# A sparse expert layer: the next tile's rows turned behind the upper block of the expert rows instead of ahead of it

## The chip, the cores and the metric

The kernel runs on one core of a Trainium2 chip. The metric is the device time of one execution in microseconds (us); three runs were timed. One further execution was profiled, and all rows below are from it.

## The reference

Three layers follow one another on 1536 tokens of 512 values: a bucketed attention, a dense mixture of experts, and a sparse mixture of experts. The change touches the third alone. There each token goes to the one expert whose embedding fits best, and its row is scaled by the probability of that choice:

```python
logits = xn @ en.T / tau
expert_idx = np.argmax(logits, axis=1)
probs = softmax(logits)
gate_w = probs[np.arange(N), expert_idx]
for e in range(E):                      # E = 8
    mask = expert_idx == e
    h = np.maximum(x[mask] @ w1[e], 0.0)        # 512 -> 1024
    out[mask] = gate_w[mask, None] * (h @ w2[e])  # 1024 -> 512
```

## The kernel before

Every fp32 operand of a large product is kept as two parts: a rounded one ("hi") and the rest ("lo"). matmul_x3 makes a product from three matmuls, hi by lo, hi by hi and lo by hi (lines L478, L479, L480). A cast on ScalarE makes hi, a subtraction on VectorE makes lo.

The sparse layer works in tiles of up to 128 tokens of one expert. A loop with a count known only at run time (tiles2) runs over the tiles of each expert, and the experts follow in order; tile numbers run through. Each engine has its own copy of this loop, written out by hand, and works strictly in its written order; semaphores alone tie the engines together. There is no scheduler.

What happens for tile i, by names of the code:

- GpSimd gathers the token rows into x_row (L656) and later stores y_row by a list of rows (L665). The gather for a later tile waits until PE has turned the x_row before it (s_xrow_t).
- PE, turn_row (L1104): four 128x128 transposes of x_row into PSUM bank 2. ScalarE, x_hi (L1341), then VectorE, x_lo (L1836), split the bank. They are done one tile ahead, for tile i + 1.
- PE, up part: for each of two column blocks c of 512, 12 matmuls into bank c. VectorE's relu (L1861) writes block c of g_row. turn_h(i, c) (L1113) turns it by four transposes into bank 6 + c; ScalarE's copy (L1361) makes g_hi of it, VectorE's g_lo (L1865) the rest. The lower block is c = 0, the upper one c = 1. turn_h(i, 0) stands inside the up part of c = 1.
- PE, down part: for f = 0 to 7, three matmuls into bank 4; f below 4 needs the lower block of g, f from 4 on the upper.
- ScalarE's y_tile (L1351) scales bank 4 into y_row.

Beside this the weights of the next expert are split: w2_hi2 (L1294) and w2_lo (L1726, called "second" in the loop) in each tile of the expert, w1_hi2 (L1289) and w1_lo2 (L1720) behind its last tile. SP loads weights when the raw buffers are free.

Of the kernel before, what the change touches and what calls it, by code (L numbers as in the profile page):

```python
# [27 lines left out]
def program(nc, q, k, v, proj, w_gate, w1, w2, emb, tau, m2w1, m2w2, out):  # L28
# [8 lines left out]
    KD, KF = DM // P, FF // P  # L37
# [14 lines left out]
    def place(name, shape, dt, at=None):  # L52
        size = 2 if dt == BF16 else 4
        for n in shape[1:]:
            size *= n
        here = top if at is None else at
        t = nc.alloc_sbuf_tensor_at(name, shape, dt, offset=here[0])
        here[0] += (size + 31) // 32 * 32
        assert here[0] <= nc.sbuf_usable_end, name
        return t  # L60
# [80 lines left out]
    w2_raw_of = [place("w2_raw_even", [P, KF, DM], F32, small), w2_raw]  # L141
# [334 lines left out]
    def matmul_x3(pe, acc, a, b, start, stop):  # L476

        pe.matmul(acc, a[0], b[1], start=start, stop=False)  # L478
        pe.matmul(acc, a[0], b[0], start=False, stop=False)  # L479
        return pe.matmul(acc, a[1], b[0], start=False, stop=stop)  # L480
# [233 lines left out]
    def _(pe):  # L714
# [385 lines left out]
        def turn_row(i):  # L1100

            pe.wait_ge(s_xrow, 16 * i + 16)
            for kd in range(KD):
                tr = pe.transpose(psum[:, 2, kd * P:(kd + 1) * P], x_row[:, kd * P:(kd + 1) * P], ident[:])  # L1104
            tr.then_inc(s_xrow_t, 1)

        def turn_h(i, c):

            pe.wait_ge(s_relu2, 2 * i + c + 3)
            pe.wait_ge(s_g_lo, 2 * i + c + 1)  # L1110
            for j in range(4):
                f = 4 * c + j
                tr = pe.transpose(psum[:, 6 + c, j * P:(j + 1) * P], g_row[:, f * P:(f + 1) * P], ident[:])  # L1113
            tr.then_inc(s_g_t, 1)

        def tiles2(e, u, first, end, more=True):
            with pe.Fori(first, end) as i:
                pe.wait_ge(s_x_lo, i + 1)
                for c in range(2):
                    pe.wait_ge(s_relu2, 2 * i + c + 1)  # L1120
                    for kd in range(KD):
                        if c == 0:
                            pe.wait_ge(m2.w1_lo, KD * e + kd + 1)
                        if c == 1 and kd == 2:
                            turn_h(i, 0)
                        mm = matmul_x3(pe, psum[:, c, :], [x[:, kd, :] for x in x_s],
                                       [w[:, kd, c * 512:(c + 1) * 512] for w in w1_s], kd == 0, kd == KD - 1)
                    mm.then_inc(s_up2, 1)
                turn_row(i + 1)
                pe.wait_ge(m2.w2_lo, KF * (i + 1) if more else KF * (first + 1))  # L1130
                pe.wait_ge(s_y2, i + 1)
                for f in range(KF):
                    if f % 4 == 0:
                        pe.wait_ge(s_g_lo, 2 * i + f // 4 + 3)
                    if f == 1:
                        turn_h(i, 1)
                    mm = matmul_x3(pe, psum[:, 4, :], [g[:, f, :] for g in g_s], [w[f] for w in w2_p[u]],
                                   f == 0, f == KF - 1)
                mm.then_inc(s_down2, 1)

        tiles2(0, 0, 0, first_end)
        with pe.Fori(0, E // 2 - 1) as e2:
            for u in (1, 0):
                e = 2 * e2 + 2 - u
                tiles2(e, u, *tile_range(pe, e))
        tiles2(E - 1, 1, *tile_range(pe, E - 1), more=False)


    @block.scalar
    def _(act):  # L1150
# [135 lines left out]
        def w1_hi2(e, raw, kds=range(KD)):  # L1286
            act.wait_ge(m2.w1_in, 16 * e + 16)
            for kd in kds:
                act.copy(w1_s[0][:, kd, :], raw[:, kd, :]).then_inc(m2.w1_hi, 1)  # L1289

        def w2_hi2(e, u, raw, fs):
            act.wait_ge(m2.w2_in, 16 * e + 16)
            for f in fs:
                act.copy(w2_p[u][0][f], raw[:, f, :]).then_inc(m2.w2_hi, 1)  # L1294
# [44 lines left out]
        def x_hi(i):  # L1339
            act.wait_ge(s_xrow_t, i + 1)  # L1340
            act.copy(x_s[0][:].rearrange("p k i -> p (k i)"), psum[:, 2, :]).then_inc(s_x_hi, 1)  # L1341
# [5 lines left out]
        def y_tile(i):  # L1347

            act.wait_ge(s_down2, i + 1)
            act.wait_ge(s_y_free, i + 1)  # L1350
            act.activation(y_row[:], psum[:, 4, :], ACT.Copy, scale=p_now[:, 0:1]).then_inc(s_y2, 1)  # L1351

        def tiles2(e, u, first, end, more=True):
            with act.Fori(first, end) as i:
                y_tile(i)
                if more:
                    act.wait_ge(m2.w2_lo, KF * (i + 1))
                    w2_hi2(e + 1, 1 - u, w2_raw_of[1 - u], range(0, KF - 1))
                for c in range(2):
                    act.wait_ge(s_g_t, 2 * i + c + 1)  # L1360
                    act.copy(g_s[0][:, 4 * c:4 * c + 4, :].rearrange("p f i -> p (f i)"),  # L1361
                             psum[:, 6 + c, :]).then_inc(s_g_hi, 1)
                    if c == 0:
                        if more:
                            w2_hi2(e + 1, 1 - u, w2_raw_of[1 - u], (KF - 1,))
                        x_hi(i + 1)
            if more:
                w1_hi2(e + 1, w1_raw_of[1 - u])

# [4 lines left out]
        first_end = act.value_load(start_i[0:1, 1:2], min_val=1, max_val=SLOTS)  # L1374
        act.wait_ge(s_x_lo, 1)
        tiles2(0, 0, 0, first_end)
        with act.Fori(0, E // 2 - 1) as e2:
            for u in (1, 0):
                e = 2 * e2 + 2 - u
                tiles2(e, u, *tile_range(act, e))  # L1380
        tiles2(E - 1, 1, *tile_range(act, E - 1), more=False)
        every = act.value_load(start_i[0:1, E:E + 1], min_val=E, max_val=SLOTS)
        y_tile(every)
# [3 lines left out]
    def _(dve):  # L1387
# [329 lines left out]
        def w1_lo2(e, raw, kds=range(KD)):  # L1717
            for kd in kds:
                dve.wait_ge(m2.w1_hi, KD * e + kd + 1)
                dve.tensor_tensor(w1_s[1][:, kd, :], raw[:, kd, :], w1_s[0][:, kd, :].bitcast(F32),  # L1720
                                  ALU.subtract).then_inc(m2.w1_lo, 1)

        def w2_lo(done, u, raw, f):

            dve.wait_ge(m2.w2_hi, done + f + 1)
            dve.tensor_tensor(w2_p[u][1][f], raw[:, f, :], w2_p[u][0][f].bitcast(F32), ALU.subtract).then_inc(m2.w2_lo, 1)  # L1726
# [107 lines left out]
        def x_lo(i):  # L1834
            dve.wait_ge(s_x_hi, i + 1)
            dve.tensor_tensor(x_s[1][:].rearrange("p k i -> p (k i)"), psum[:, 2, :],  # L1836
                              x_s[0][:].rearrange("p k i -> p (k i)").bitcast(F32), ALU.subtract).then_inc(s_x_lo, 1)
# [21 lines left out]
        def relu(i, c):  # L1859
            dve.wait_ge(s_up2, 2 * i + c + 1)  # L1860
            dve.tensor_scalar(g_row[:, c * 512:(c + 1) * 512], psum[:, c, :], 0.0, None, ALU.max).then_inc(s_relu2, 1)  # L1861

        def g_lo(i, c):
            dve.wait_ge(s_g_hi, 2 * i + c + 1)
            dve.tensor_tensor(g_s[1][:, 4 * c:4 * c + 4, :].rearrange("p f i -> p (f i)"), psum[:, 6 + c, :],  # L1865
                              g_s[0][:, 4 * c:4 * c + 4, :].rearrange("p f i -> p (f i)").bitcast(F32),
                              ALU.subtract).then_inc(s_g_lo, 1)

        def tiles2(e, u, first, end, more=True):
            with dve.Fori(first, end) as i:  # L1870

                def second(*fs):
                    if more:
                        for f in fs:
                            w2_lo(KF * (i + 1), 1 - u, w2_raw_of[1 - u], f)

                second(0, 1)
                relu(i, 0)
                second(2, 3, 4)
                g_lo(i, 0)  # L1880
                relu(i, 1)
                second(5)
                x_lo(i + 1)
                second(6)
                g_lo(i, 1)
                second(7)
            if more:
                w1_lo2(e + 1, w1_raw_of[1 - u])

        tiles2(0, 0, 0, first_end)  # L1890
        with dve.Fori(0, E // 2 - 1) as e2:
            for u in (1, 0):
                e = 2 * e2 + 2 - u
                tiles2(e, u, *tile_range(dve, e))
        tiles2(E - 1, 1, *tile_range(dve, E - 1), more=False)

    block.__exit__(None, None, None)
# [28 lines left out]
```

## Time and profile before

| | us |
|---|---|
| median of 3 runs | 1570.8 (1570.76 to 1570.91) |
| profiled execution | 1570.51 |
| its span | 1568.6 |
| PE busy | 1545.6 (99%) |
| PE weight loads busy | 1292.6 (82%) |
| VectorE busy | 686.0 (44%) |
| ScalarE busy | 516.0 (33%) |
| GpSimd busy | 332.3 (21%) |

The chain that ended last is PE for 96% of the span. The sparse layer's tiles lie between 1346 and 1560 us. A matmul of 512 columns is listed with some 0.39 us, but the next one starts 0.23 us behind it: matmuls overlap, and their pitch is what counts. PEld rows are the weight loads that go ahead of each matmul. Around each row stand the start, the length, the engine, the line and the tiles, and in brackets the idle time before it with what ended it.

### The profile page before, as it was taken

What the parts mean: (1) busy time and instruction counts of PE and PEld (TensorE: products, weight loads), DVE (VectorE), ACT (ScalarE), POOL (GpSimd) and SP (SyncE); (2) the same over time, 40 slices, a digit from 0 to 9 for tenths busy, and PEclk for the clock granted to TensorE, in tenths of its full rate; (3) what the DMA queues carried; (4) which work ended last, traced back from release to release, by engine and by line L of the source; (5) the groups of instructions that cost most, each with busy time, mean ns of one, the idle gap of its engine ahead of it and who ended that gap; (6) DMA issues with size and microseconds to landing.
All of it is one profiled execution on the core that took longest, in us unless ns stands there. A gap on an engine that the chain in (4) does not pass through costs nothing.

```text
span 1568.6 us, 21673 instructions
## 1 busy us (share of the span) xinstructions
PE 1545.6 (99%) x7493; PEld 1292.6 (82%) x7494; DVE 686.0 (44%) x1242; ACT 516.0 (33%) x946; POOL 332.3 (21%) x563
## 2 busy tenths in 40 slices
PE   8999999999999999999999999999999999999997
PEld 7999997888888888888888888888888888788886
DVE  7999985423222311311322221121132255887665
ACT  6888885012111101101211111011121133676554
POOL 4565656000300300120030030012004000233222
PEclk9999999999999999999999999999999999899999
DMA  6545561101100200110110011011011122774310
GB/s 164 136 113 144 124 179 55 54 1 54 55 1 1 80 27 0 53 53 0 53 54 0 0 68 39 0 53 53 0 38 69 41 81 75 251 260 163 118 40 25
DMA packets 44775, 108.88 MB, mean 69 GB/s; under 512 B 5782, under 2 KB 7830, under 8 KB 44736
## 3 DMA queue, kind: packets, MB, share of 16 engines
q1 hardware_dynamic: 41088, 99.83, 20.4%
q0 software_dynamic: 3424, 8.14, 1.6%
q8 instruction: 24, 0.39, 0.1%
q10 hardware_dynamic: 224, 0.39, 0.1%
q14 instruction: 15, 0.12, 0.0%
HBM read 81.57 MB, written 8.13 MB: 57 GB/s over the span
## 4 chain that ended last, share of the span: by engine, by line
PE 96%; DVE 2%; ACT 1%; issue 1%; POOL 0%; DVEq 0%; POOLq 0%; ACTq 0%
PE psum L478 27%; PE psum L479 26%; PE psum L480 26%; PE psum L786 4%; PE psum L773 2%; PE psum L800 2%; PE psum L799 2%; PE psum L774 2%; PE psum L1113 1%; PE psum L754 1%; PE psum L813 1%; PE psum L920 1%; PE psum L1104 0%; ACT prob L1169 0%; DVE pt_lo L1431 0%
## 5 line engine op out<-in xcount | busy, mean ns | idle before, releaser
L1302 ACT ACTIVATE h_hi<-psum 128x512 fp32r<-128x512 f32 x192 | 114.9, 598 | 878.5 <-PE psum L480 878.5
L478 PE MATMUL psum<-w_lo,h_hi 128*128 128x512 f32 x768 | 304.4, 396 | 0.0
L479 PE MATMUL psum<-w_hi,h_hi 128*128 128x512 f32 x768 | 302.5, 394 | 0.0
L478 PE MATMUL psum<-xt_lo,w_hi 128*128 128x512 f32 x768 | 300.3, 391 | 0.0
L479 PE MATMUL psum<-xt_hi,w_hi 128*128 128x512 f32 x768 | 299.0, 389 | 0.0
L480 PE MATMUL psum<-xt_hi,w_lo 128*128 128x512 f32 x768 | 298.9, 389 | 0.0
L480 PE MATMUL psum<-w_hi,h_lo 128*128 128x512 f32 x768 | 298.5, 389 | 0.0
L1737 DVE SCALAR_TENSOR_TENSOR h_lo<-psum,h_hi 128x512 fp32r<-128x512 f32 x192 | 133.0, 693 | 351.3 <-ACT h_hi L1302 351.3
L1800 DVE SCALAR_TENSOR_TENSOR tok<-psum,route,tok 128x512 f32<-128x512 f32 x83 | 56.8, 745 | 358.6 <-PE psum L480 358.6
L509 POOL CAST w_hi<-w_raw 128x512 fp32r<-128x512 f32 x68 | 41.6, 611 | 802.0 <-PE psum L480 801.6
L480 PEld LDWEIGHTS psum<-w_hi,h_lo 128*128 128x128 f32 x768 | 144.2, 188 | 32.5
L478 PEld LDWEIGHTS psum<-w_lo,h_hi 128*128 128x128 f32 x768 | 144.2, 188 | 32.1
L480 PEld LDWEIGHTS psum<-xt_hi,w_lo 128*128 128x128 f32 x768 | 144.2, 188 | 30.1
L478 PEld LDWEIGHTS psum<-xt_lo,w_hi 128*128 128x128 f32 x768 | 144.2, 188 | 29.8
L479 PEld LDWEIGHTS psum<-xt_hi,w_hi 128*128 128x128 f32 x768 | 144.2, 188 | 29.4
L479 PEld LDWEIGHTS psum<-w_hi,h_hi 128*128 128x128 f32 x768 | 144.6, 188 | 27.4
L1431 DVE TENSOR_TENSOR pt_lo<-psum,pt_hi 128x384 fp32r<-128x384 f32 x192 | 97.5, 549 | 18.4 <-ACT pt_hi L1162 17.7
L1169 ACT ACTIVATE prob<-psum,row_bias,row_scale 128x768 f32<-128x768 f32 x96 | 95.9, 999 | 20.4 <-POOL row_bias L558 18.6
L1441 DVE TENSOR_REDUCE row_min<-psum 128x1 f32<-128x768 f32 x96 | 90.8, 947 | 1.1 <-PE psum L774 0.7
L1162 ACT CAST pt_hi<-psum 128x384 fp32r<-128x384 f32 x192 | 83.0, 486 | 14.1 <-PE psum L786 12.9
L631 POOL TENSOR_TENSOR w_lo<-w_raw,w_hi 128x512 fp32r<-128x512 f32 x64 | 82.6, 1291 | 12.5 <-issue 7.2
L786 PE MATMUL psum<-ident,prob 128*128 128x128 f32 x576 | 80.7, 275 | 2.2 <-DVE pt_lo L1431 1.7
(272 smaller groups left out, 1996.0 us busy)
## 6 DMA issues: line engine op xcount, KB each, us to landing
w_raw<-in_moe_w_dram SPq DMA_DIRECT2D x25, 2048.0 KB, 8.2
w_raw_odd<-in_moe_w_dram SPq DMA_DIRECT2D x4, 2048.0 KB, 10.3
k_hh<-k_hi SPq DMA_DIRECT2D x32, 192.0 KB, 3.0
w_raw_even<-in_moe_w_dram SPq DMA_DIRECT2D x3, 2048.0 KB, 9.2
x_rows<-tok SPq DMA_DIRECT2D x14, 256.0 KB, 2.4
k_raw<-in_k_dram SPq DMA_DIRECT2D x8, 384.0 KB, 3.1
v_raw<-in_v_dram SPq DMA_DIRECT2D x16, 192.0 KB, 3.4
q_b<-q_hi SPq DMA_DIRECT2D x16, 192.0 KB, 4.0
```

The lines of the kernel that those rows point to most:

```text
L478: pe.matmul(acc, a[0], b[1], start=start, stop=False)
L479: pe.matmul(acc, a[0], b[0], start=False, stop=False)
L480: return pe.matmul(acc, a[1], b[0], start=False, stop=stop)
L631: pool.tensor_tensor(w2_s[1][:, f, :], w2_raw[:, f, :], w2_s[0][:, f, :].bitcast(F32), ALU.subtract).then_inc(m1.w2_lo, 1)
L786: tr = pe.transpose(psum[:, 4 + c, j * P:j * P + P], prob[par][:, 3 * c + j, :], ident[:])
L1162: act.copy(pt_hi[half][:, 3 * c:3 * c + 3, a:a + P], psum[:, 4 + c, 0:HALF].rearrange("p (j i) -> p j i", j=3)).then_inc((s_hi_a, s_hi_b)[ ...
L1169: act.activation(prob[t % 2][:].rearrange("p (c j) i -> p c (j i)", c=2), psum[:, score_bank(g, t):score_bank(g, t) + 2, 0:HALF], ACT.Exp, ...
L1302: act.activation(h_s[0][:, f, :], psum[:, f % 4, :], ACT.Relu).then_inc(m1.h_hi, 1)
L1431: dve.tensor_tensor(pt_lo[half][:, 3 * c:3 * c + 3, a:a + P], psum[:, 4 + c, 0:HALF].rearrange("p (j i) -> p j i", j=3), pt_hi[half][:, 3 ...
L1441: dve.tensor_reduce(row_min[:, c], psum[:, score_bank(g, t):score_bank(g, t) + 2, 0:HALF], AX.XY, ALU.min).then_inc(s_min, 1)
L1737: dve.scalar_tensor_tensor(h_s[1][:, f, :], psum[:, f % 4, :], 0.0, h_s[0][:, f, :].bitcast(F32), ALU.max, ALU.subtract).then_inc(m1.h_lo, 1)
L1800: dve.scalar_tensor_tensor(tok[:, tile, 0:DM], psum[:, 4 + i, :], route[:, e, tile:tile + 1], tok[:, tile, 0:DM], ALU.mult, ALU.add).then_ ...
```

## The change

In PE's loop, turn_row(i + 1) goes from between the up part and the down part to behind turn_h(i, 1), which stands behind the three matmuls of f = 0. ScalarE makes x_hi(i + 1) behind the copies of both blocks instead of behind that of the lower one. VectorE makes g_lo(i, 1) before x_lo(i + 1), and second(6) ahead of both. Nothing is added or left out.

```diff
@@ PE, tiles2
                     mm.then_inc(s_up2, 1)
-                turn_row(i + 1)
                 pe.wait_ge(m2.w2_lo, KF * (i + 1) if more else KF * (first + 1))
                 pe.wait_ge(s_y2, i + 1)
                 for f in range(KF):
                     if f % 4 == 0:
                         pe.wait_ge(s_g_lo, 2 * i + f // 4 + 3)
                     if f == 1:
                         turn_h(i, 1)
+                        turn_row(i + 1)
@@ ScalarE, tiles2
                     act.copy(g_s[0][:, 4 * c:4 * c + 4, :].rearrange("p f i -> p (f i)"),
                              psum[:, 6 + c, :]).then_inc(s_g_hi, 1)
-                    if c == 0:
-                        if more:
-                            w2_hi2(e + 1, 1 - u, w2_raw_of[1 - u], (KF - 1,))
-                        x_hi(i + 1)
+                    if c == 0 and more:
+                        w2_hi2(e + 1, 1 - u, w2_raw_of[1 - u], (KF - 1,))
+                x_hi(i + 1)
@@ VectorE, tiles2
                 relu(i, 1)
-                second(5)
+                second(5, 6)
+                g_lo(i, 1)
                 x_lo(i + 1)
-                second(6)
-                g_lo(i, 1)
                 second(7)
```

PE at the end of the up part of a tile (w_hi and w_lo are w1, xt_hi and xt_lo hold w2 here, ISA and REGISTER_ALU prepare a wait), before:

```order
L480 MATMUL psum<-w_hi,x_lo 128x512
L1102 ISA
L1104 MATMUL psum<-ident,x_row 128x128 x4
L1130 REGISTER_ALU
L478 MATMUL psum<-xt_lo,g_hi 128x512
L479 MATMUL psum<-xt_hi,g_hi 128x512
L480 MATMUL psum<-xt_hi,g_lo 128x512
L1109 REGISTER_ALU
L1113 MATMUL psum<-ident,g_row 128x128 x4
L478 MATMUL psum<-xt_lo,g_hi 128x512
```

The same place on PE with the change:

```order
L480 MATMUL psum<-w_hi,x_lo 128x512
L1129 REGISTER_ALU
L478 MATMUL psum<-xt_lo,g_hi 128x512
L479 MATMUL psum<-xt_hi,g_hi 128x512
L480 MATMUL psum<-xt_hi,g_lo 128x512
L1109 REGISTER_ALU
L1113 MATMUL psum<-ident,g_row 128x128 x4
L1102 ISA
L1104 MATMUL psum<-ident,x_row 128x128 x4
L478 MATMUL psum<-xt_lo,g_hi 128x512
```

The four transposes of x_row have moved past three matmuls and past the four transposes of g_row.

VectorE from the upper relu to the end of the tile (L1726 is "second"), before:

```order
L1861 TENSOR_SCALAR g_row<-psum 128x512
L1725 REGISTER_ALU
L1726 TENSOR_TENSOR w_lo<-w_raw,w_hi 128x512
L1835 REGISTER_ALU
L1836 TENSOR_TENSOR x_lo<-psum,x_hi 128x512
L1725 REGISTER_ALU
L1726 TENSOR_TENSOR w_lo<-w_raw,w_hi 128x512
L1865 TENSOR_TENSOR g_lo<-psum,g_hi 128x512
L1725 REGISTER_ALU
L1726 TENSOR_TENSOR w_lo<-w_raw,w_hi 128x512
```

The same place on VectorE with the change (its lines stand one lower in number):

```order
L1860 TENSOR_SCALAR g_row<-psum 128x512
L1724 REGISTER_ALU
L1725 TENSOR_TENSOR w_lo<-w_raw,w_hi 128x512
L1724 REGISTER_ALU
L1725 TENSOR_TENSOR w_lo<-w_raw,w_hi 128x512
L1864 TENSOR_TENSOR g_lo<-psum,g_hi 128x512
L1834 REGISTER_ALU
L1835 TENSOR_TENSOR x_lo<-psum,x_hi 128x512
L1724 REGISTER_ALU
L1725 TENSOR_TENSOR w_lo<-w_raw,w_hi 128x512
```

x_lo has moved behind a w2 rest and g_lo.

## Rows read from the trace of the kernel before

**Rows 1.** Stretches: length, busy us (instructions) per engine, PEclk, DMA share, GB/s.

```profile
1340.00:1346.00 6.00, 4.25 (x21) 3.21 (x21) 3.96 (x20) 2.28 (x4) 0.90 (x5) 0.63 0.63 241
1346.00:1352.00 6.00, 6.00 (x15) 4.69 (x16) 2.97 (x9) 4.59 (x9) 2.40 (x3) 0.52 0.22 54
...
1429.17:1441.52 12.35, 12.35 (x61) 10.19 (x60) 8.12 (x14) 6.60 (x13) 3.32 (x4) 1.00 0.13 43
1441.52:1454.02 12.50, 12.50 (x62) 10.12 (x61) 12.42 (x18) 10.39 (x17) 4.31 (x4) 1.00 0.62 198
```

**Rows 2.** Waits from 1346 us on: who for whom, total us, times, longest.

```profile
POOL x_row L656 <- PE psum L1104: 52.2, 17, 5.1
...
POOL out_dram L665 <- POOL idx_now L509: 3.0, 3, 1.0
...
PEld psum L478 <- DVE w_lo L1720: 2.0, 7, 0.3
...
PE psum L478 <- DVE x_lo L1840: 0.4, 1, 0.4
```

**Rows 3.** Timeline of the weight loads in one tile: start, length, engine, line, operation.

```profile
1429.17 0.59 PEld L1104 LDWEIGHTS psum<-ident,x_row 128*128 128x128 f32 x4
...
1430.08 0.19 PEld L480 LDWEIGHTS psum<-xt_hi,g_lo 128*128 128x128 f32 x1
1430.35 0.56 PEld L1113 LDWEIGHTS psum<-ident,g_row 128*128 128x128 f32 x4
...
1430.98 0.19 PEld L479 LDWEIGHTS psum<-xt_hi,g_hi 128*128 128x128 f32 x1
...
1432.83 0.19 PEld L478 LDWEIGHTS psum<-xt_lo,g_hi 128*128 128x128 f32 x1
```

**Rows 4.** Timeline of PE in the same tile.

```profile
1429.17 0.39 PE L480 MATMUL psum<-w_hi,x_lo 128*128 128x512 f32 x1
1429.40 0.60 PE L1104 MATMUL psum<-ident,x_row 128*128 128x128 f32 x4
...
1430.54 0.60 PE L1113 MATMUL psum<-ident,g_row 128*128 128x128 f32 x4
```

**Rows 5.** Timeline of VectorE in the same tile.

```profile
1428.83 0.69 DVE L1865 TENSOR_TENSOR g_lo<-psum,g_hi 128x512 fp32r<-128x512 f32 x1
1429.60 0.69 DVE L1861 TENSOR_SCALAR g_row<-psum 128x512 f32<-128x512 f32 x1
1430.21 0.68 DVE L1726 TENSOR_TENSOR w_lo<-w_raw,w_hi 128x512 fp32r<-128x512 f32 x1
...
1432.01 0.69 DVE L1865 TENSOR_TENSOR g_lo<-psum,g_hi 128x512 fp32r<-128x512 f32 x1
1432.61 0.68 DVE L1726 TENSOR_TENSOR w_lo<-w_raw,w_hi 128x512 fp32r<-128x512 f32 x1
```

**Rows 6.** All instructions of line L1861: ns shortest/median/longest, first and last start.

```profile
L1861 DVE TENSOR_SCALAR g_row<-psum x34: 678/692/694, 1351.5 to 1553.5; 128x512 f32<-128x512 f32 x34
```

**Rows 7.** Timeline of the weight loads behind a change of the expert.

```profile
1413.04 0.19 PEld L478 LDWEIGHTS psum<-w_lo,x_hi 128*128 128x128 f32 x1 [0.31 <-DVE w_lo L1720]
1413.15 0.19 PEld L479 LDWEIGHTS psum<-w_hi,x_hi 128*128 128x128 f32 x1
1413.39 0.19 PEld L480 LDWEIGHTS psum<-w_hi,x_lo 128*128 128x128 f32 x1
```

**Rows 8.** Timeline of ScalarE in the tile of rows 3.

```profile
1430.04 0.59 ACT L1341 CAST x_hi<-psum 128x512 fp32r<-128x512 f32 x1 [0.72 <-PE psum L1104]
1431.18 0.59 ACT L1361 CAST g_hi<-psum 128x512 fp32r<-128x512 f32 x1 [0.55 <-PE psum L1113]
```

**Rows 9.** Timeline of GpSimd around the change to the third and fourth tile.

```profile
1387.41 0.78 POOL L509 COPY idx_now<-tab 128x3 uint32 x1 [5.37 <-DMA x_row<-x_rows,idx_now]
...
1393.60 0.94 POOL L656 DMA_INDIRECT x_row<-x_rows,idx_now  x1 [1.53 <-PE psum L1104]
```

## The prediction

> **What bounds the kernel now.** I read four views in this order: the table of stretches for two whole tiles of the sparse layer, the table of waits over that layer, the start times on PE, its weight loads, VectorE and ScalarE around one tile's boundary between upper and lower block, and last GpSimd, because the moved step also releases a gather.
>
> PE is busy 12.35 of 12.35 us in one tile and 12.50 of 12.50 in another [rows 1]. From 1346 us on only one wait of PE for another engine is listed, 0.4 us for the first x_lo; its weight loads waited 2.0 us in seven places for L1720 [rows 2]. So the sparse layer is a dense row of PE work. An added PE instruction or wait lengthens it, and other engines matter only when PE reaches something they have not finished.
>
> The place of the change is the end of the up part. Let T0 be the start of its last matmul, 1429.17 [rows 4]. The weight load of turn_row starts at T0 too, its first transpose at 1429.40 = T0+0.23 [rows 3, 4]. VectorE finishes g_lo of the lower half at 1428.83+0.69 = 1429.52 = T0+0.35, and begins relu of the upper half at 1429.60 = T0+0.43, which is done at 1430.29 = T0+1.12 [rows 5]. turn_h(i, 1) needs that relu: its weight load starts at 1430.35 = T0+1.18, 0.06 us after relu's end. Without a wait it would have started one matmul behind the load at 1430.08, at 1430.31 [rows 3]. It is therefore already held back by 0.04 us, which is not seen on PE, since its first transpose runs at 1430.54 = T0+1.37, one matmul pitch (0.23) after 1430.31 [rows 4]. The reader is to see that turn_row lies exactly in the shadow in which relu is made, and that nothing of this shadow is left over. relu takes 678 to 694 ns in all 34 cases [rows 6], so there is no tile in which it is shorter.
>
> **The change part by part.** Nothing is added or removed in count: per tile four transposes, one CAST and one TENSOR_TENSOR change places.
>
> (a) PE. Four transposes keep their price: the weight load of the next matmul stands at 1430.98, the first transpose at 1430.54, so 0.44 us for four, 0.11 each [rows 3, 4]. Behind turn_h they cost 0.44 again. Ahead of it they no longer cost it if the three matmuls of f = 0 could run at once.
>
> They can't. The load of f = 0 would want to start at T0, but it waits for g_lo of the lower half, ready at T0+0.35, so about T0+0.40 (with the 0.06 seen between relu and its waiter, T0+0.41). A late load shows at the change of an expert, where PE waits for L1720: load at 1413.04, the next load (which starts with the late matmul) at 1413.15, the one after at 1413.39 [rows 7]. So the late matmul runs 0.11 us after its load, the second 0.35. The f = 0 matmuls start at T0+0.52, 0.76, 0.99, and turn_h could run at T0+1.22.
>
> relu holds it further. Its end does not move: it hangs on the last up matmul, which stays at T0. The load of turn_h is released at T0+1.18, its first transpose runs at T0+1.29. Then eight transposes at 0.11 end at T0+2.17; before, the matmul of f = 1 came at T0+1.37+0.44 = T0+1.81. Loss: 0.36 us a tile, for 17 tiles (34 relus, two a tile [rows 6]) 6.1 us. Said otherwise: 0.44 moved out of the shadow, less 0.08 because turn_h starts that much sooner.
>
> Bounds of this unknown. A gain is no end of the range, since PE's work stays and it waited for nothing here before. The trace shows no late load of this kind before a transpose. Lower end: if the transpose started at once with its load, the loss would be 0.36-0.11 = 0.25, 4.3 us. Upper end: if it had to wait the full 0.19 of a load, 0.44, and if the two register and wait instructions between turn_h and turn_row, which after a stall are not fetched ahead, cost another 0.06 (the distance from a release to its waiter), 0.50, 8.5 us. I take 0.36, from the only late load in the rows.
>
> The Trainium skill, page "TensorE: Matmul & The Clock Gate", section "Architectural detail: the array is 16× 32×32, not 1× 128×128", says that a matmul can begin before its weight load completes. By that rule the sum stays at 6.1; by a reading in which the load of 0.19 us must be complete it would be 17 x 0.44 = 7.5. The late load of [rows 7] agrees with the rule: 0.11 against 0.19.
>
> (b) The upper half's own chain. g_hi begins 0.64 us behind the first transpose (1430.54 to 1431.18 [rows 4, 8]), now at T0+1.93, done at T0+2.52. g_lo, no longer behind x_lo, starts at T0+2.57 instead of 1432.01 = T0+2.84 [rows 5] and is done at T0+3.26. PE's load for f = 4 stood at 1432.83 = T0+3.66 [rows 3] against g_lo's end at T0+3.53; it moves to T0+4.02. The slack grows from 0.13 to 0.76 us, worth nothing, as PE was not waiting there: at 1432.83 the load runs on time.
>
> (c) The x chain. x_hi follows g_hi on ScalarE, done about T0+3.1; x_lo starts one VectorE pitch (1429.60 to 1430.21, 0.6 us [rows 5]) behind g_lo, at T0+3.17, and ends at T0+3.86. The next tile needs it about T0+6.8 (21 matmuls at a pitch of 0.23 behind T0+2.17, less a pitch by which the load is ahead). Hidden by three microseconds of down matmuls. Without that cover each late 0.1 would cost 0.1.
>
> (d) The change of an expert. The fourth rest w_lo of the next w1 was too late in seven places (2.0 us of waiting loads [rows 2]); in time each costs 0.15 us (a tile of 12.50 instead of 12.35 [rows 1]), 1.0 us in all. VectorE reaches these rests one pitch behind its last w2 rest, which stood at 1432.61 = T0+3.44 [rows 5] and now stands at T0+3.77: 0.33 later, while PE comes 0.36 later. Gain 0.03 each, 0.2 us. w1_hi moves 0.5 to 0.6 us later on ScalarE but stays ahead of VectorE.
>
> (e) GpSimd. The gather of the next rows waits for turn_row: 52.2 us of waiting in 17 cases [rows 2]. turn_row starts at T0+1.73 instead of T0+0.23, so the gather goes 1.5 us later. Hidden behind the same wait, with what stands under the third rival. SP's loads follow w_lo and move by 0.3.
>
> Sum: 6.1-0.2 = +5.9 us against the profiled execution's 1570.51 (span 1568.6), so 1576.4. The median of the runs is 1570.8, 0.3 above; forecast 1576.7, +0.38%. Changes within 0.2% (3.1 us) can't be told from none.
>
> **Rivals.**
> Not slower: PE finds relu ready. Were turn_h's load really held by PE's own order and the 0.04 us a chance, the transposes would only change places, and instead the late w_lo at the expert changes would be all that moves: PE's 7 x 0.15 = 1.0 us may go, 1569.8. It decides in this way if turn_h's load can start by T0+0.80. For it speaks that no row names relu as releaser of PE. Against: relu ends at T0+1.12 and starts with the last matmul's result, 0.43 behind T0. Chance 0.06.
>
> The clock falls. PE would now stand idle 0.36 us in each tile. In 1340 to 1346 us, with PE busy 4.25 of 6, the granted clock was 0.63, and 0.52, nearly all of it at the lower level of 1.2 GHz, in the 6 us behind, where 15 matmuls ran in 6.0 us, 2.6 us more than at a pitch of 0.23 [rows 1]. One more such stretch gives 1579.3, one in each tile 1621. Against: the idle share would be 3%, not 29%. Chance 0.03. The Trainium skill, "TensorE: Matmul & The Clock Gate", section "A second HAM failure mode: psum-queue depth-cycling", says that frequent micro-idles between groups of matmuls can make the clock oscillate; no row here shows it at idle gaps this short.
>
> GpSimd becomes late. Where weights are being loaded, the gathered rows kept the next step waiting 5.37 us, and the gather of the next tile then waited only 1.53 for PE [rows 9]; in three tiles the store went straight behind idx_now [rows 2]. 1.5 us more makes store, p_now and y_row of these tiles late; ScalarE does y_row, seven casts and then g_hi, so PE would wait for g_lo. If 1 us of it reached PE in three tiles, 1579.7. Against: after a delay of 1.5 the next gather's release is 1.5 later too. Chance 0.07.
>
> **Chances.** Forecast 0.82 (its own range 1574.9 to 1579.1 from the bounds in (a)), not slower 0.06, clock 0.03, GpSimd 0.07, else 0.02. Range 1574.3 to 1579.9, which reaches from a little below the forecast's range to the GpSimd case. Faster by over 0.2%: 0.02; within: 0.07; slower: 0.91.
>
> **What would show it.** Tiles of 12.71 and about 12.83 us instead of 12.35 and 12.50; two listed waits of PE's loads per tile, for g_lo L1864 and relu L1860; turn_h's load 0.06 us behind relu's end; eight transposes in a row at 0.11; g_lo at T0+2.57. I am wrong if the load of f = 0 starts at T0, if turn_h's starts before T0+1.1, or if a tile grows by under 0.25 or over 0.50 us.

## The result and the profile after

Six runs of the changed kernel have a median of 1576.99 us (1576.77 to 1578.34), six of the kernel before on the same chip 1570.92 (1570.76 to 1571.13): 6.07 us more, ratio 1.004 with a 95% interval of 1.0029 to 1.005. The forecast was 1576.7. The profiled span is 1575.0 us against 1568.6.

To keep the sparse layer apart from what runs ahead of it, I take T0 (the start of the last up matmul) of the first and of the last of its 17 tiles from the timelines: 1354.48 and 1553.08 before, 1354.73 and 1559.14 after. The 16 tiles between them take 198.60 and 204.41 us, so 5.81 more or 0.363 a tile. The same loss behind the last T0 makes 6.2; the other 0.25 of the span's 6.4 lies ahead of the first T0, where nothing was changed. In the profiles of all kernels below the first T0 lies anywhere between 1353.21 and 1355.92, so the 16 tiles tell small differences better than the run times.

The stretches of two tiles, one in the middle of an expert and one behind a change of expert, with length, busy us per engine in the order PE, PEld, VectorE, ScalarE, GpSimd, granted clock, DMA share and GB/s:

```profile
1380.42:1393.29 12.87, 12.71 (x62) 10.08 (x60) 12.51 (x18) 10.29 (x17) 3.79 (x4) 1.00 0.96 366
1482.72:1495.41 12.69, 12.59 (x61) 10.11 (x60) 8.20 (x14) 6.50 (x13) 3.32 (x4) 1.00 0.13 41
```

Where PE was busy for the whole tile before [rows 1], it now is not, and the granted clock stays at 1.00. The idle time is smaller than the loss, because the row of a matmul is listed with 0.39 us while its pitch is 0.23. Waits in the sparse layer of the changed kernel, as who for whom, us in all, times, longest:

```profile
POOL x_row L656 <- PE psum L1104: 62.6, 14, 4.8
POOL x_row L656 <- DMA out_dram<-y_row,idx_now: 14.4, 3, 4.9
...
PEld psum L478 <- issue: 8.2, 16, 0.6
...
PEld psum L1113 <- DVE g_row L1860: 2.0, 11, 0.2
PEld psum L478 <- DVE w_lo L1719: 1.7, 7, 0.2
PEld psum L478 <- DVE xt_lo L1725: 1.4, 2, 0.7
PE psum L478 <- DVE g_lo L1864: 1.1, 5, 0.3
```

Of the waits of PE and its loads in this list [rows 2] had only the one for w_lo, of 2.0 us. The new ones have to be read with the code beside them: "issue" (but for one of 0.4 us that the kernel before had as well) and "xt_lo" both stand at the first load of f = 0, which the code lets wait for the lower g_lo. The view names no releaser, or the wrong one, because that g_lo had ended 0.12 us before the load began. One tile shows it; first the weight loads (start, length, engine, line):

```profile
1431.45 0.19 PEld L480 LDWEIGHTS psum<-w_hi,x_lo 128*128 128x128 f32 x1
1432.15 0.19 PEld L478 LDWEIGHTS psum<-xt_lo,g_hi 128*128 128x128 f32 x1 [0.51 <-issue]
1432.26 0.19 PEld L479 LDWEIGHTS psum<-xt_hi,g_hi 128*128 128x128 f32 x1
1432.50 0.19 PEld L480 LDWEIGHTS psum<-xt_hi,g_lo 128*128 128x128 f32 x1
1432.85 0.47 PEld L1113 LDWEIGHTS psum<-ident,g_row 128*128 128x128 f32 x4 [0.17 <-DVE g_row L1860]
1433.29 0.47 PEld L1104 LDWEIGHTS psum<-ident,x_row 128*128 128x128 f32 x4
...
1433.83 0.19 PEld L479 LDWEIGHTS psum<-xt_hi,g_hi 128*128 128x128 f32 x1
...
1435.68 0.19 PEld L478 LDWEIGHTS psum<-xt_lo,g_hi 128*128 128x128 f32 x1
```

PE in the same tile:

```profile
1431.68 0.39 PE L480 MATMUL psum<-w_hi,x_lo 128*128 128x512 f32 x1
1432.18 0.47 PE L478 MATMUL psum<-xt_lo,g_hi 128*128 128x512 f32 x1
1432.49 0.39 PE L479 MATMUL psum<-xt_hi,g_hi 128*128 128x512 f32 x1
...
1432.96 0.60 PE L1113 MATMUL psum<-ident,g_row 128*128 128x128 f32 x4
1433.39 0.60 PE L1104 MATMUL psum<-ident,x_row 128*128 128x128 f32 x4
```

VectorE:

```profile
1431.34 0.69 DVE L1864 TENSOR_TENSOR g_lo<-psum,g_hi 128x512 fp32r<-128x512 f32 x1
1432.10 0.69 DVE L1860 TENSOR_SCALAR g_row<-psum 128x512 f32<-128x512 f32 x1
1432.71 1.28 DVE L1725 TENSOR_TENSOR w_lo<-w_raw,w_hi 128x512 fp32r<-128x512 f32 x2
1434.21 0.69 DVE L1864 TENSOR_TENSOR g_lo<-psum,g_hi 128x512 fp32r<-128x512 f32 x1 [0.22 <-ACT g_hi L1361]
1434.82 0.68 DVE L1835 TENSOR_TENSOR x_lo<-psum,x_hi 128x512 fp32r<-128x512 f32 x1
1435.42 0.68 DVE L1725 TENSOR_TENSOR w_lo<-w_raw,w_hi 128x512 fp32r<-128x512 f32 x1
```

Here T0 is 1431.68. The lower g_lo ends at T0+0.35, as before, and relu at T0+1.11, as before [rows 5]: neither has moved. PE has: its f = 0 load waits until T0+0.47, turn_h's until T0+1.17, and the load behind f = 1's first matmul comes at T0+2.15, where it came at T0+1.81 [rows 3]. turn_h starts 0.09 us sooner than before [rows 4], and 0.43 to 0.44 of turn_row now follow it.

Two loads wait in this tile, but only one of the waits holds PE. The first transpose of turn_h, 1432.96, stands 0.47 us behind the second matmul of f = 0, 1432.49. That is two pitches of 0.23, as in a row without a gap. In all 17 tiles this distance is 0.46 to 0.48, in the 11 where a wait for relu is listed and in the 6 where none is. So turn_h's load waited for relu while PE still had matmuls to run, and the lower g_lo alone sets the time.

### The profile page after: what moved, and what is told of

It is laid out like the page before. It is cut to its first block, busy times and chain, and to the rows that moved or that the text cites. A ratio compares the mean times of both kernels' runs of the same rounds, so it can differ in the third digit from the quotient of the medians.

```text
span 1575.0 us, 21673 instructions
## 1 busy us (share of the span) xinstructions
PE 1549.4 (98%) x7493; PEld 1291.4 (82%) x7494; DVE 687.2 (44%) x1242; ACT 514.2 (33%) x946; POOL 329.9 (21%) x563
## 4 chain that ended last, share of the span: by engine, by line
PE 93%; DVE 3%; issue 2%; ACT 1%; DVEq 0%; DMA 0%; POOL 0%; ACTq 0%; POOLq 0%
PE psum L478 26%; PE psum L479 25%; PE psum L480 25%; PE psum L786 4%; PE psum L773 2%; PE psum L800 2%; PE psum L799 2%; PE psum L774 2%; PE psum L1113 1%; PE psum L754 1%; PE psum L813 1%; PE psum L920 1%; DVE xt_lo L1725 0%; DVE w_lo L1725 0%; PE psum L1104 0%
```

## The experiments

All times are medians beside runs of the kernel before on the same chip, whose median there was 1569.5 to 1571.1. "16 tiles" is the stretch from the first T0 to the last, "tile" the common distance of two T0 within an expert and over a change of expert, all from the timelines.

| kernel | time (before) | ratio, 95% interval | 16 tiles | tile within / at a change |
|---|---|---|---|---|
| before | | | 198.60 | 12.34 / 12.50 |
| changed | 1576.99 (1570.92) | 1.0040 (1.0029 to 1.0050) | 204.41 | 12.69 / 12.79 to 12.90 |
| PE's move alone | 1591.25 (1571.05) | 1.0129 (1.0112 to 1.0146) | 218.57 | 13.51 / 13.85 |
| ScalarE and VectorE alone | 1573.11 (1571.05) | 1.0014 (1.0005 to 1.0024) | 201.60 | 12.35 / 12.89 |
| changed, filler in the old place | 1578.15 (1571.05) | 1.0048 (1.0032 to 1.0065) | 205.64 | 12.80 / 12.89 |
| before, one transpose of four | 1570.33 (1571.05) | 0.9995 (0.9985 to 1.0005) | 198.16 | 12.26 / 12.51 |
| before, filler behind turn_row | 1577.22 (1571.13) | 1.0041 (1.0025 to 1.0056) | 204.62 | 12.78 / 12.79 |
| changed, turns behind f = 1 | 1582.19 (1571.13) | 1.0074 (1.0059 to 1.0089) | 209.28 | 12.70 / 13.50 |
| before, w1_lo last | 1570.55 (1571.13) | 0.9997 (0.9988 to 1.0006) | 198.17 | 12.35 / 12.35 |
| changed, lower turn earlier | 1577.50 (1569.47) | 1.0043 (1.0027 to 1.0060) | 204.25 | 12.66 / 12.76 to 12.92 |
| both earlier | 1582.03 (1569.47) | 1.0076 (1.0059 to 1.0093) | 208.70 | 12.66 / 13.26 to 13.61 |
| lower rest freed | 1577.97 (1570.78), one run | | 205.55 | 12.65 / 13.10 |
| both freed | 1576.02 (1570.78), one run | | 205.01 | 12.46 / 13.25 |

**The two halves of the change.** PE's move alone:

```diff
-                turn_row(i + 1)
...
                     if f == 1:
                         turn_h(i, 1)
+                        turn_row(i + 1)
```

> The kernel before with PE's part of the change alone: turn_row behind turn_h(i, 1), while ScalarE still makes x_hi before the upper g_hi and VectorE x_lo before the upper g_lo. Theory (the shadow of relu and of the lower g_lo is lost): 0.36 us a tile as in the whole change, and on top the upper g_lo comes late: x_hi from T0+2.35, x_lo 2.99, a w2 rest 3.59, g_lo 4.19 to 4.88, PE's load for f = 4 at T0+4.93 instead of 4.02, 0.79 more a tile; tiles of about 13.5 us, some 21 us over before, about 1592. Rival (the order on ScalarE and VectorE is worth nothing, PE alone decides): as the whole change, 1577.

Measured 1591.25 and tiles of 13.51. Waits of that kernel:

```profile
PEld psum L478 <- DVE g_lo L1865: 15.6, 17, 1.0
...
PE psum L478 <- DVE g_lo L1865: 8.4, 16, 0.5
```

The upper g_lo (L1865) is now waited for by PE's load of f = 4 in every tile. The theory's term for it holds (12.70+0.79 = 13.49). So the new order on ScalarE and VectorE is worth some 14 us to this PE order, though it saves nothing against the kernel before.

The change on ScalarE and VectorE alone, with turn_row in its old place:

```diff
-                    if c == 0:
-                        if more:
-                            w2_hi2(e + 1, 1 - u, w2_raw_of[1 - u], (KF - 1,))
-                        x_hi(i + 1)
+                    if c == 0 and more:
+                        w2_hi2(e + 1, 1 - u, w2_raw_of[1 - u], (KF - 1,))
+                x_hi(i + 1)
...
-                second(5)
-                x_lo(i + 1)
-                second(6)
-                g_lo(i, 1)
+                second(5, 6)
+                g_lo(i, 1)
+                x_lo(i + 1)
```

> The change on ScalarE and VectorE alone, PE's order as before. Theory: PE's stretch at the block boundary stays at 12.34 us a tile, since turn_row fills the shadow again; but VectorE now idles until the upper g_hi is done and reaches the rests of the next w1 at T0+4.45 instead of T0+4.03, so each of the seven late changes of an expert costs 0.42 us more: 1573.8. Rival 1 (the loss of the whole change lies in these two engines): 1577. Rival 2 (their order is worth nothing): 1570.9.

Tiles within an expert stay at 12.35, but for two of 12.45 and 12.46 whose lower g_lo ends as late as T0+0.53 and T0+0.56; those at a change grow from 12.50 to 12.89, the 16 tiles by 3.0 us. The run times, 2.1 us more, agree within their interval (0.8 to 3.8 us). PE waits for the same instruction as before, the rest of the next w1, only longer and more often [rows 2]:

```profile
PEld psum L478 <- DVE w_lo L1719: 5.9, 14, 0.6
PE psum L478 <- DVE w_lo L1719: 1.2, 7, 0.2
```

Within an expert, then, all of the change's loss comes with PE's move.

**How long is the open stretch?** Four transposes are put where turn_row stood, in the changed kernel and behind turn_row in the kernel before:

```diff
+        def filler():
+            for j in range(4):
+                pe.transpose(psum[:, 3, j * P:(j + 1) * P], ident[:], ident[:])
...
+                filler()
                 pe.wait_ge(m2.w2_lo, KF * (i + 1) if more else KF * (first + 1))
```

> The changed kernel with four more transposes (of the identity, into a PSUM bank that nobody reads) where turn_row stood before. They are added work of PE that is no part of the result. Theory (a shadow of 0.36 us stands open there): the four cost only 0.44-0.36 = 0.08 us a tile, turn_h starts at T0+1.37 again; tiles of 12.78 instead of 12.70; 1577.6 to 1578.3. Rival (the loss comes from eight transposes in a row or from the moved instructions themselves, not from an open shadow): 0.44 us a tile more, 1584.4.

> The kernel before with four more transposes (of the identity, into a PSUM bank that nobody reads) directly behind turn_row. Theory (the shadow is full already): all 0.44 us are paid in each tile, tiles of 12.78, 7.5 us, less 1.0 because the rests of the next w1 are then no longer late: 1577.4. Rival (the shadow has room): under 1573.

In the changed kernel the filler costs 0.11 us a tile (12.80 against 12.69), or 0.08 over the 16; in the kernel before, where the stretch is full, 0.44 (12.78 against 12.34). The same four instructions cost at least four times as much there. The weight loads of the changed kernel with filler (L1118) show no listed wait around them, and turn_h's transposes start at T0+1.38, where they were before the change:

```profile
1494.64 0.59 PEld L1118 LDWEIGHTS psum<-ident 128*128 128x128 f32 x4
1495.20 0.19 PEld L478 LDWEIGHTS psum<-w_lo,g_hi 128*128 128x128 f32 x1
...
1495.82 0.56 PEld L1113 LDWEIGHTS psum<-ident,g_row 128*128 128x128 f32 x4
1496.35 0.47 PEld L1104 LDWEIGHTS psum<-ident,x_row 128*128 128x128 f32 x4
```

The opposite test takes three of turn_row's four transposes out of the kernel before, so that most rows of the sparse layer are stale:

```diff
-            for kd in range(KD):
+            for kd in range(1):
                 tr = pe.transpose(psum[:, 2, kd * P:(kd + 1) * P], x_row[:, kd * P:(kd + 1) * P], ident[:])
```

> The kernel before with turn_row cut to the first of its four transposes, in the old place; three quarters of the next tile's rows are not turned, so most of the sparse layer's input is stale. Theory (0.36 us of the 0.44 lie in the shadow): f = 0 waits for the lower g_lo until T0+0.41, turn_h for relu, its first transpose at T0+1.29; a tile wins 0.08 us, 12.26, and the late w1 rests give some of it back: 1569.5 to 1570.1. Rival (PE's work is what counts): three transposes of 0.11 gone, 0.33 a tile, 1565.3.

Tiles of 12.26: three of four transposes gone bring 0.08 us, not 0.33. At the changes of expert this comes back (12.51), and the run time can't be told from before.

**Which of the two waits?** In the changed kernel turn_h and turn_row are put behind f = 1:

```diff
-                    if f == 1:
+                    if f == 2:
                         turn_h(i, 1)
                         turn_row(i + 1)
```

> The changed kernel with turn_h(i, 1) and turn_row one f later, behind the matmuls of f = 1, so that relu is done when turn_h comes. Theory (two waits lie one behind the other): PE still waits for the lower g_lo, 0.29 us a tile, tiles of 12.63 within an expert; the upper chain moves 0.6 us later, so the next w1 rests come at T0+4.99 and a change of the expert costs some 0.67 more: 1579 to 1581. Rival (relu is the only wait): tiles of 12.34 within an expert.

The rival falls: with relu out of the way the tiles still take 12.70. No wait of L1113 is listed any more, and the one for the lower g_lo is unchanged:

```profile
PEld psum L478 <- issue: 8.2, 16, 0.6
```

But 12.63 was expected too. The expectation let f = 0 load at T0+0.41; it loads at T0+0.47, and PE's row goes on from T0+0.58 instead of T0+0.23. So this wait alone costs 0.35, the whole loss. At a change of expert PE's loads wait 7.6 us in all for w1's rests instead of 1.7, which makes the tiles of 13.50 and a time above the 1579 to 1581 expected. The next experiment makes g_lo's wait shorter in the changed kernel by turning the lower block one matmul sooner:

```diff
+                        if c == 1 and kd == 1:
+                            part = [w[:, kd, c * 512:(c + 1) * 512] for w in w1_s]
+                            pe.matmul(psum[:, c, :], x_s[0][:, kd, :], part[1], start=False, stop=False)
+                            pe.matmul(psum[:, c, :], x_s[0][:, kd, :], part[0], start=False, stop=False)
+                            turn_h(i, 0)
+                            pe.matmul(psum[:, c, :], x_s[1][:, kd, :], part[0], start=False, stop=False)
+                            continue
-                        if c == 1 and kd == 2:
-                            turn_h(i, 0)
```

> The changed kernel with turn_h(i, 0) one matmul earlier in the up part (ahead of the third matmul of kd = 1 instead of ahead of kd = 2), so that the lower g_lo is done about T0+0.15 instead of T0+0.35. Theory (the wait for g_lo and the one for relu end at the same point, either alone costs the tile its 0.35 us): relu takes over, its waits grow from 0.19 to about 0.4, and tiles within an expert stay at 12.69; the whole 1577 to 1578. Rival (the wait for g_lo is the whole cost): tiles of 12.49.

The same with the turns behind f = 1:

> The same with turn_h(i, 1) and turn_row behind the matmuls of f = 1 as well, so that relu is done in time. Theory: only what is left of the wait for g_lo stays, its first matmul at T0+0.38 instead of T0+0.23, so 0.15 us: tiles within an expert of 12.49; the changes of an expert cost more, as with the turns behind f = 1 alone. Rival (the cost is in the eight transposes or in the new place of the turns, not in the waits): 12.69 again.

Both missed their premise. g_lo still stood behind three w2 rests in VectorE's row and ended at T0+0.32 instead of T0+0.35, so the first can't be counted as a hit. The tiles follow those 0.03 us in both (12.66), with relu in the way and without. Only the first and the last of the 17 tiles show the full effect. The last has no rests; its loads with the lower turn earlier:

```profile
1560.19 0.19 PEld L478 LDWEIGHTS psum<-w_lo,g_hi 128*128 128x128 f32 x1 [0.28 <-issue]
...
1561.13 0.42 PEld L1113 LDWEIGHTS psum<-ident,g_row 128*128 128x128 f32 x4 [0.40 <-DVE g_row L1865]
```

So the two were run again, with one w2 rest moved behind relu:

```diff
-                second(2, 3, 4)
+                second(2, 3)
                 g_lo(i, 0)
                 relu(i, 1)
-                second(5, 6)
+                second(4, 5, 6)
```

> As with the lower turn earlier, and on VectorE one of the three w2 rests ahead of the lower g_lo put behind relu, since those three kept g_lo at its old time in every tile but the last (that tile has no rests to make, and there the wait for g_lo fell from 0.50 to 0.28 us while that for relu rose from 0.18 to 0.40). Theory (either wait alone costs nearly all of it): now in all tiles within an expert relu takes over; tiles of 12.64 to 12.69. Rival (g_lo's wait is the whole cost): 12.49.

> The same with turn_h(i, 1) and turn_row behind the matmuls of f = 1. Theory: both waits are relieved together, tiles within an expert of 12.46 to 12.49; changes of an expert stay dear, since the next w1 rests come later still. Rival (the new place of the turns costs by itself): no tile under 12.60.

Now the lower g_lo ends at T0+0.11 to 0.13 in all tiles, and the waits split cleanly. With the turns behind f = 0, loads and matmuls of one tile (T0 = 1495.99):

```profile
1496.23 0.19 PEld L478 LDWEIGHTS psum<-w_lo,g_hi 128*128 128x128 f32 x1 [0.28 <-issue]
...
1497.16 0.42 PEld L1113 LDWEIGHTS psum<-ident,g_row 128*128 128x128 f32 x4 [0.40 <-DVE g_row L1865]
```

```profile
1496.57 0.40 PE L479 MATMUL psum<-w_hi,g_hi 128*128 128x512 f32 x1
...
1497.16 0.66 PE L1113 MATMUL psum<-ident,g_row 128*128 128x128 f32 x4
1497.66 0.60 PE L1104 MATMUL psum<-ident,x_row 128*128 128x128 f32 x4
```

Here turn_h comes 0.59 us behind the second matmul of f = 0 and no longer 0.46 to 0.48: relu has taken over.

With the turns behind f = 1:

```profile
1494.68 0.19 PEld L478 LDWEIGHTS psum<-w_lo,g_hi 128*128 128x128 f32 x1 [0.27 <-issue]
...
1495.94 0.59 PEld L1113 LDWEIGHTS psum<-ident,g_row 128*128 128x128 f32 x4
```

| | g_lo as it was | g_lo 0.2 sooner |
|---|---|---|
| turns behind f = 0 (relu not ready) | 12.69 | 12.65 |
| turns behind f = 1 (relu ready) | 12.70 | 12.46 |

Relieving g_lo's wait alone brings 0.04, because relu then takes over; taking relu away alone brings nothing; both together bring 0.23. What is left of 12.46 over 12.34 is the rest of g_lo's wait: f = 0 loads at T0+0.24, and the next load, at T0+0.34 to 0.35, is 0.12 late. So the turns' new place costs nothing by itself. The tiles at a change of expert lose instead: with the rest moved behind relu and the turns behind f = 0, the waiting of PE's loads for w1's rests grows from 1.7 to 4.1 us, and the tiles to 13.10. The run times of these two kernels, one each, settle nothing; the tiles do.

**The late rests at a change of expert.** In the kernel before, the matmul with the last w1_lo comes last of its three:

```diff
+                        if c == 0 and kd == KD - 1:
+                            acc, part = psum[:, c, :], [w[:, kd, c * 512:(c + 1) * 512] for w in w1_s]
+                            pe.wait_ge(m2.w1_hi, KD * e + kd + 1)
+                            pe.matmul(acc, x_s[0][:, kd, :], part[0], start=False, stop=False)
+                            pe.matmul(acc, x_s[1][:, kd, :], part[0], start=False, stop=False)
+                            pe.wait_ge(m2.w1_lo, KD * e + kd + 1)
+                            mm = pe.matmul(acc, x_s[0][:, kd, :], part[1], start=False, stop=True)
+                            continue
```

> The kernel before, but in the up part's lower column block the product of the fourth 128 rows takes its two matmuls with w1_hi first and the one with w1_lo last, and waits for w1_lo only ahead of that one. Theory (0.15 us in each of seven changes of an expert are a wait for the last w1 rest): they go, tiles of 12.34 throughout, 1569.8. Rival (12.50 has another cause, such as the loop's turn): 1570.9.

The 12.50 become 12.35 in five of seven cases, as forecast (12.41 and 12.45 in the other two), but the 16 tiles win only 0.43 of the 1.0 us. Other tiles grow: the one with its T0 at 1391.91 takes 12.52, where 12.35 stood. VectorE and the load of f = 0 there:

```profile
1391.83 0.68 DVE L1873 TENSOR_TENSOR g_lo<-psum,g_hi 128x512 fp32r<-128x512 f32 x1
```

```profile
1391.91 0.59 PEld L1104 LDWEIGHTS psum<-ident,x_row 128*128 128x128 f32 x4
1392.62 0.19 PEld L478 LDWEIGHTS psum<-w_lo,g_hi 128*128 128x128 f32 x1
```

g_lo ends at 1392.51, and f = 0 waits for it even behind turn_row. VectorE is busy for 12.42 of 12.50 us of a tile at a change of expert [rows 1]; the backlog that PE no longer waits for at w1 reaches it at g_lo. Of the kernels that compute everything this one has the shortest 16 tiles, but in run time it can't be told from before.

## Why the prediction was right, point by point

- **The shadow behind the up part, 0.36 us a tile, 6.1 us.** Right in size: 12.69 against 12.34, and 0.363 a tile over the 16, 0.36 forecast. Shown by both fillers, the quarter turn and the halves of the change.
- **Which wait makes it.** Wrong; the size came out by luck. The forecast let PE's row go on from T0+0.52, so that turn_h would be free at T0+1.22, and then "relu holds it further", to T0+1.29. In the runs turn_h was free at T0+1.27 and relu held it no further. Two terms were mis-sized against each other. The step "it waits for g_lo, so about T0+0.40" gave this wait the 0.06 between end and waiter that relu has; the rows show 0.11 to 0.12, and f = 0's load came at T0+0.47. And relu alone would have let turn_h go at T0+1.23, as the kernel with the lower rest freed shows (turn_row's first transpose at T0+1.67, less 0.44). The loss stayed the same because the two limits lie 0.04 us apart. Of the two listed waits a tile that the prediction names as its sign, relu's stands in 11 of 17 tiles and g_lo's under other names.
- **A late weight load costs 0.11.** Right for the matmuls of f = 0: load at 1432.15, and the next load, which starts with the late matmul, at 1432.26. (The matmul's own row begins at 1432.18 but is 0.47 long instead of 0.39, and the next one begins at 1432.49, a pitch behind 1432.26.) Too much for transposes: in the kernel with the lower rest freed the load comes at 1497.16 and turn_row's first transpose at 1497.66, 0.50 behind; less four at 0.11 that leaves 0.06. The 0.11 from 1432.85 to 1432.96 is not its price, since PE could not have turned sooner. The bound with a full load of 0.19 is excluded. So are 0.06 more for waits between the turns, since turn_row's first transpose follows at 0.43 to 0.44; that instructions there are not fetched ahead, as this bound supposed, no run shows.
- **The upper half's chain.** g_lo at T0+2.53 (forecast 2.57), x_lo at T0+3.14 (3.17), the load of f = 4 at T0+4.00 (4.02). Worth nothing against the kernel before, as said; that it was worth 14 us against PE's move alone the prediction did not work out.
- **The change of an expert.** Too simple. The w1 rests did about what was forecast: the waiting loads fell from 2.0 to 1.7 us. But tiles at a change took 12.79 to 12.90 where about 12.83 was forecast, and two within an expert 12.86 and 12.87 where 12.71 was. The prediction took the lower g_lo to end at T0+0.35 everywhere. In six tiles it is later by VectorE's own row. In the worst two, weight loads and VectorE of the changed kernel look like this (T0 = 1393.29):

```profile
1393.93 0.19 PEld L478 LDWEIGHTS psum<-w_lo,g_hi 128*128 128x128 f32 x1 [0.69 <-DVE xt_lo L1725]
```

```profile
1390.73 0.68 DVE L1860 TENSOR_SCALAR g_row<-psum 128x512 f32<-128x512 f32 x1
1391.33 1.89 DVE L1725 TENSOR_TENSOR xt_lo<-w_raw_even,xt_hi 128x512 fp32r<-128x512 f32 x3
1393.13 0.68 DVE L1864 TENSOR_TENSOR g_lo<-psum,g_hi 128x512 fp32r<-128x512 f32 x1
```

  Five instructions without a gap end in g_lo at T0+0.52 instead of T0+0.35, and PE's load comes at T0+0.64 instead of T0+0.47. In the kernel before g_lo was late in the same six tiles (T0+0.37 to 0.44), but turn_row covered it: there f = 0 loads at T0+0.56 in any case. Now turn_h starts at T0+1.31 to 1.45 in these six, and at 1.26 to 1.29 in the other eleven. Added up, that is some 0.6 us that the prediction lacks. The sum of 5.9 thus came out close partly by luck as well: 17 tiles at 0.34 (T0+2.15 instead of T0+1.81) in place of 0.36 are 0.3 less, the late g_lo 0.6 more.
- **GpSimd.** The gather moved by 1.5 us, and in three tiles it then had the store's landing to wait for instead of PE (14.4 us in the waits above). None of it delayed ScalarE's y_row: y_row's waits are for PE in all 17 cases, as before.
- **The rivals.** Not slower: excluded by the time and by turn_h's load at T0+1.17. The clock: the granted clock from 1356 to 1564 us is 1.00 in the changed kernel and in every other kernel here. GpSimd: not seen.

## What to carry to other kernels

Work that stands between a producer's last matmul and the first wait for its result is paid for by that wait; before moving it, measure the shadow from the producer to the end of each result that is waited for behind it, and take the later of them. Take the distance from a result's end to its waiter from the same place; it was not the same for two results here. On an engine that is busy throughout, moved work costs what the old place hid, less what the new place starts sooner, and a filler of known price in the old place measures that directly. A listed wait of a weight load need not hold the matmuls: look whether they still follow at their pitch. Where two waits end almost at the same point, relieving one shows little: test them crosswise.

## What the runs showed of the hardware that was not expected

The load of f = 0 starts 0.11 to 0.12 us behind the end of the g_lo that it waits for (1432.03 to 1432.15; 1393.81 to 1393.93; 1392.51 to 1392.62), that of turn_h mostly 0.05 to 0.06 behind relu (1432.79 to 1432.85). Ahead of f = 0 the code has three waits, ahead of turn_h two; whether that is the reason was not tried and stays open.

A load that came late held a matmul of 512 columns back by 0.11 us (1432.15 to 1432.26) and a row of 128-column transposes by 0.06 (1497.16, with the fifth transpose at 1497.66). Why the two differ was not tried either.
